# Expert layer: rows kept in token order, tiles gathered and scattered by row number on GpSimd

## What is computed

```python
# 1. banded attention, 8 heads of 64; keys: the first 8, and the last 96 up to the query
scores = q @ k.T / 8 - slope[h] * dist ;  a = softmax(scores where kept) ;  x = a @ v
# 2. one of 8 experts per token
logits = x @ w_gate ; gate = sigmoid(x @ w_local)
for s in tokens of a batch:
    e = argmax(logits[s]) if s == 0 or gate[s] < 0.5 else previous e
    out[s] = softmax(logits[s])[e] * (relu(x[s] @ w1[e]) @ w2[e])   # w1[e] 512x1024, w2[e] 1024x512
# 3. rotation and mixing
theta = x @ w_theta ; zr, zi = x * cos(theta), x * sin(theta)
u = x + w_tok_r @ zr + w_tok_i @ zi ;  result = u + relu(u @ w_ch)
```

## Time and profile before

| what | us |
|---|---|
| median of three executions | 620.63 |
| lowest and highest | 617.61 and 622.44 |
| the profiled execution | 617.87 |
| its span, first to last instruction | 616.2 |
| share of the span that TensorE is busy | 85% |
| mean granted TensorE clock | 0.934 of full speed |

### The profile page before, as it was taken

One profiled execution on the slowest core, in us unless ns is written; L12 is line 12 of the kernel. 1 busy time (PEld: TensorE's weight loads), 2 busy tenths in 40 slices (PEclk: granted clock), 3 DMA queues, 4 the chain that ended last, 5 costly groups with the idle time before them and its releaser, 6 DMA issues.

```text
span 616.2 us, 9126 instructions
## 1 busy us (share of the span) xinstructions
PE 522.7 (85%) x3252; PEld 430.0 (70%) x3253; DVE 282.8 (46%) x606; ACT 202.6 (33%) x420; POOL 116.4 (19%) x116
## 2 busy tenths in 40 slices
PE   0788888887502999999998999984799999999987
PEld 0566666664202999989997988973578887888866
DVE  5456565552332214141425144114789768655234
ACT  1466657651120113131334133113454423232011
POOL 4655555501043002020122020007100000000000
PEclk9998878898855999999999999996799999999999
DMA  5634434556023404572939564005200000000002
GB/s 196 219 127 137 132 131 133 173 248 277 1 106 132 170 34 182 227 286 106 374 104 398 247 238 171 34 26 152 61 0 2 1 1 1 17 18 18 35 34 87
DMA packets 22563, 77.61 MB, mean 126 GB/s; under 512 B 3456, under 2 KB 3712, under 8 KB 18432
## 3 DMA queue, kind: packets, MB, share of 16 engines
q0 software_dynamic: 8032, 46.67, 19.4%
q1 hardware_dynamic: 11904, 26.31, 12.8%
q10 hardware_dynamic: 2592, 4.20, 2.0%
HBM read 61.43 MB, written 15.73 MB: 125 GB/s over the span
## 4 chain that ended last, share of the span: by engine, by line
PE 59%; issue 17%; DVE 8%; DMA 6%; POOL 5%; ACT 3%; SPq 1%; DVEq 0%; POOLq 0%; ACTq 0%
PE ps L1154 33%; PE ps L1179 10%; POOL k_lo L452 4%; PE ps L998 3%; PE ps L1053 3%; PE ps L1037 3%; DMA q_raw<-in_q 3%; DMA w_sb<-in_w_experts 2%; PE ps L1115 2%; PE ps L1107 1%; POOL q_lo L447 1%; PE ps L1240 1%; PE ps L1018 1%; DVE w_lo L877 1%; PE ps L1165 1%
## 5 line engine op out<-in xcount | busy, mean ns | idle before, releaser
L1179 PEld LDWEIGHTS ps<-xT,w_sb 128*128 128x128 f32 x1024 | 118.0, 194 | 5.4 <-issue 3.0
L1179 PE MATMUL ps<-xT,w_sb 128*128 128x128 f32 x1024 | 118.5, 277 | 3.2 <-DMA w_sb<-in_w_experts 2.2
L868 DVE SCALAR_TENSOR_TENSOR hT_lo<-ps,hT_hi 128x512 fp32r<-128x512 f32 x32 | 21.8, 689 | 97.8 <-ACT hT_hi L576 97.6
L877 DVE TENSOR_TENSOR w_lo<-w_sb,w_hi 128x1024 fp32r<-128x1024 f32 x32 | 37.0, 1220 | 47.4 <-ACT w_hi L589 47.4
L1154 PE MATMUL ps<-w_hi,hT_hi 128*128 128x512 f32 x128 | 51.4, 401 | 2.2 <-DVE hT_lo L868 2.2
L525 ACT ACTIVATE prob<-raw,row_min 128x256 f32<-128x256 f32 (+1 forms) x96 | 46.0, 483 | 18.7 <-DVE row_min L736 18.6
L1154 PE MATMUL ps<-w_hi,hT_lo 128*128 128x512 f32 x128 | 50.0, 391 | 0.0
L1154 PE MATMUL ps<-w_lo,hT_hi 128*128 128x512 f32 x128 | 49.9, 390 | 0.0
L998 PE MATMUL ps<-k_hi,q_hi 64*128 64x256 f32 (+1 forms) x96 | 21.5, 441 | 31.5 <-POOL k_lo L452 30.1
L464 POOL DMA_DIRECT2D w_sb<-in_w_experts x32 | 17.3, 543 | 159.9 <-PE ps L1154 141.2
L576 ACT ACTIVATE hT_hi<-ps 128x512 fp32r<-128x512 f32 x32 | 19.0, 595 | 84.6 <-PE ps L1179 84.6
(11 more groups left out here) (184 smaller groups left out, 1009.0 us busy)
## 6 DMA issues: line engine op xcount, KB each, us to landing
w_sb<-in_w_experts POOLq DMA_DIRECT2D x32, 1024.0 KB, 9.1
v_sb<-in_vx SPq DMA_DIRECT2D x8, 640.0 KB, 5.1
slots<-zero SPq DMA_DIRECT2D x20, 256.0 KB, 5.2
xin<-slots SPq DMA_DIRECT2D x17, 256.0 KB, 2.6
slots<-yout ACTq DMA_DIRECT2D x16, 256.0 KB, 2.7
k_raw<-in_kx SPq DMA_DIRECT2D x8, 432.0 KB, 6.1
q_raw<-in_q SPq DMA_DIRECT2D x8, 384.0 KB, 6.5
out_x<-o_sb SPq DMA_DIRECT2D x12, 256.0 KB, 2.0
```

The source lines that it names most:

```text
L868: dve.scalar_tensor_tensor(hT_lo[:, part, :], ps[:, 1 + half, :].rearrange("p (c q) -> p c q", c=4), 0.0, hT_hi[:, part, :].bitcast(F32), ...
L877: dve.tensor_tensor(quarter(w_lo, par, q), quarter(w_sb, par, q), w2_hi_quarter(q).bitcast(F32), ALU.subtract).then_inc(s_w2_lo, 1)
L1179: last = pe.matmul(ps[:, 1 + half, f * P:(f + 1) * P], w_sb[:, par, c // 2, j:j + P], xT[:, c, :], start=(c == 0), stop=(c == DC - 1))
```

## The change

`slots` and its zero fill are gone. The tokens are stored in `x_rows` in token order, by two plain stores on SP as soon as attention is through. From the slots, VectorE and TensorE build the inverse map `token_at`: for each tile, one row number per partition (an out-of-range number where no token stands, which the DMA leaves out). GpSimd gathers each tile's rows from `x_rows` by these numbers, and scatters each result tile to `y_rows`. The loads of weights move from GpSimd's queue to SP's, ScalarE's store goes to GpSimd as a scatter, and the last gather becomes 12 plain loads on SP.

```diff
-                for t in (2 * h, 2 * h + 1):
-                    sp.dma_start(slots[t], zero[:]).then_inc(s_zero_out, 16)
...
+            sp.wait_ge(s_x_done, 1)
+            expert_weights(0, 0)
+            sp.wait_ge(s_x_done, PAIRS // GROUP)
+            for b in range(B):
+                sp.dma_start(x_rows.rearrange("(b i p) d -> b p i d", b=B, p=P)[b],
+                             x_tok[:, b * QT:(b + 1) * QT, :]).then_inc(s_x_out, 16)
+            expert_weights(1, 1)
...
+            with sp.Fori(0, E // 2 - 1) as pair:
+                for par in range(2):
+                    done = sp.value_load(first_tile[0:1, bass.ds(2 * pair + par + 1, 1)], min_val=1,
+                                         max_val=SLOT_TILES)
+                    sp.wait_ge(s_m_y, done + 1)
+                    expert_weights(2 * pair + par + 2, par)
...
-            with sp.Fori(0, total) as t:
-                sp.wait_ge(s_m_tx, t + 1)
-                sp.dma_start(xin[:], slots[bass.ds(t + 1, 1)].rearrange("o p d -> p (o d)")).then_inc(s_m_xin, 16)
+            sp.wait_ge(s_m_yout, 16 * total)
+            for n in range(NT):
+                sp.dma_start(x_tok[:, n, :], y_rows[n * P:(n + 1) * P, :]).then_inc(gathered[n], 16)
...
+            def rows_of(t):
+                pool.tensor_copy(rows_in[:], token_at[:, bass.ds(t + 1, 1)]).then_inc(s_row_in, 1)
+                pool.wait_ge(s_row_in, t + 1)
+                pool.sem_inc(s_row_seen, 1)
+                pool.indirect_dma_start(xin[:], None, x_rows, bass.IndirectOffsetOnAxis(ap=rows_in[:], axis=0),
+                                        bounds_check=last_row, oob_is_err=False).then_inc(s_m_xin, 16)
+
+            def store_rows(t):
+                pool.wait_ge(s_m_yev, t + 2)
+                pool.tensor_copy(rows_out[:], token_at[:, bass.ds(t + 1, 1)]).then_inc(s_row_out, 1)
+                pool.wait_ge(s_row_out, t + 1)
+                pool.sem_inc(s_row_seen, 1)
+                pool.indirect_dma_start(y_rows, bass.IndirectOffsetOnAxis(ap=rows_out[:], axis=0), yout[:], None,
+                                        bounds_check=last_row, oob_is_err=False).then_inc(s_m_yout, 16)
+
+            rows_of(0)
+            pool.wait_ge(s_m_tx, 1)
+            rows_of(1)
+            store_rows(0)
+            with pool.Fori(1, total) as t:
+                pool.wait_ge(s_m_tx, t + 1)
+                rows_of(t + 1)
+                pool.wait_ge(s_m_yout, 16 * t)
+                pool.sem_inc(s_y_free, 1)
+                store_rows(t)
...
                 act.wait_ge(s_m_y, t + 2)
-                act.wait_ge(s_m_yout, 16 * t + 16)
+                act.wait_ge(s_y_free, t + 1)
                 act.copy(yout[:], ps[:, 3, :]).then_inc(s_m_yev, 1)
-                act.wait_ge(s_m_yev, t + 2)
-                act.dma_start(slots[bass.ds(t, 1)].rearrange("o p d -> p (o d)"), yout[:]).then_inc(s_m_yout, 16)
...
-            dve.tensor_copy(slot[:], val).then_inc(s_slot_ready, 1)
+            then(dve.tensor_copy(slot[:], val))
+            dve.tensor_scalar(slot_part[:, 0, :], slot[:], 7, None, ALU.arith_shift_right).then_inc(s_slot_ready, 1)
+            then(dve.tensor_scalar(slot_part[:, 1, :], slot[:], P - 1, None, ALU.bitwise_and))
+            then(dve.tensor_copy(part_f[:], slot_part[:]))
...
+            dve.tensor_tensor(in_tile[:], con("tile").rearrange("p (n c) -> p n c", n=NT), along(part_f[:, 0, :], MAP),
+                              ALU.is_equal)
+            then(dve.tensor_tensor(at_place[:], over("place", P), along(part_f[:, 1, :], P), ALU.is_equal))
+            dve.tensor_tensor(of_tile[:], in_tile[:], along(con("token"), MAP), ALU.mult).then_inc(s_of_tile, 1)
...
+            dve.wait_ge(s_inverse, 1)
+            then(dve.tensor_scalar(found[:, 0, :], ps[:, 3, 0:MAP], 0.0, float(2 * TOKENS), ALU.is_equal, ALU.mult))
+            then(dve.scalar_tensor_tensor(found[:, 1, :], ps[:, 3, 0:MAP], 1.0, found[:, 0, :], ALU.subtract, ALU.add))
+            dve.tensor_copy(token_at[:, 1:], found[:, 1, :]).then_inc(s_map, 1)
...
+            for n in range(NT):
+                last = pe.matmul(ps[:, 3, 0:MAP], at_place[:, n, :], of_tile[:, n, :], start=(n == 0), stop=(n == NT - 1))
+            last.then_inc(s_inverse, 1)
```

More of the change, by code:

```diff
@@ L35 @@
 SLOT_TILES = (B * S - E) // P + E
+TOKENS = B * S
+MAP = SLOT_TILES + 1
 HALF = S // 2
@@ L56 @@
 _WIDTHS = [("rel", REL), ("key", S), ("ident", P), ("before", P), ("ones", P), ("first", NT), ("erev", NT * E), ("eone", NT * E), ("starts", E * NT),
-           ("carry", E * NT)]
+           ("carry", E * NT), ("place", P), ("token", NT), ("tile", NT * MAP)]
 COL, _at = {}, 0
@@ L82, in constants @@
     put("carry", np.tile(np.arange(NT) > 0, E)[None])
+    put("place", np.arange(P)[None])
+    put("token", p + np.arange(NT)[None] * P + 1)
+    put("tile", np.tile(np.arange(MAP), NT)[None])
     return t
@@ L128, in program @@
             consts, out):
-    slots = nc.dram_tensor("slots", [SLOT_TILES + 1, P, D], F32, kind="Internal").ap()
+    x_rows = nc.dram_tensor("x_rows", [TOKENS, D], F32, kind="Internal").ap()
+    y_rows = nc.dram_tensor("y_rows", [TOKENS, D], F32, kind="Internal").ap()
     with ExitStack() as ctx:
@@ L193, in program @@
         s_slot_ready = sem("slot_ready")
-        s_scattered = sem("scattered")
+        s_x_out = sem("x_out")
+        s_cleared = sem("cleared")
+        s_of_tile = sem("of_tile")
+        s_inverse = sem("inverse")
+        s_map = sem("map")
+        s_row_in = sem("row_in")
+        s_row_out = sem("row_out")
+        s_row_seen = sem("row_seen")
+        s_y_free = sem("y_free")
         s_m_xin = sem("m_xin")
@@ L253, in program @@
         half_pi = sb("half_pi", [P, 1])
-        slot = sb("slot", [P, NT], U32)
+        slot = sb("slot", [P, NT], I32)
+        token_at = sb("token_at", [P, 1 + MAP], U32)
+        rows_in = sb("rows_in", [P, 1], U32)
+        rows_out = sb("rows_out", [P, 1], U32)
         first_tile = sb("first_tile", [P, E + 1], I32)
@@ L299, in program @@
         small = sb("small", [P, 6, E])
+        slot_part = sb("slot_part", [P, 2, NT], I32)
+        part_f = sb("part_f", [P, 2, NT])
+        at_place = sb("at_place", [P, NT, P], F32R)
+        in_tile = sb("in_tile", [P, NT, MAP])
+        of_tile = sb("of_tile", [P, NT, MAP], F32R)
+        found = sb("found", [P, 2, MAP])
         end_routing = cursor[0]
@@ L411, in _ @@
                                  consts[:, key + WINDOW:key + S]).then_inc(s_rest_in, 16)
-                    sp.wait_ge(s_zeroed, 1)
-                for t in (2 * h, 2 * h + 1):
-                    sp.dma_start(slots[t], zero[:]).then_inc(s_zero_out, 16)
-            for t in range(2 * H, SLOT_TILES + 1):
-                sp.dma_start(slots[t], zero[:]).then_inc(s_zero_out, 16)
-            sp.wait_ge(s_slot_ready, 1)
-            total = sp.value_load(first_tile[0:1, E:E + 1], min_val=E, max_val=SLOT_TILES)
@@ L420, in _, with expert_weights @@
-            sp.wait_ge(s_scattered, 16 * NT)
-            sp.dma_start(xin[:], slots[0]).then_inc(s_m_xin, 16)
-            with sp.Fori(0, total) as t:
-                sp.wait_ge(s_m_tx, t + 1)
-                sp.dma_start(xin[:], slots[bass.ds(t + 1, 1)].rearrange("o p d -> p (o d)")).then_inc(s_m_xin, 16)
-            sp.wait_ge(s_m_yout, 16 * total + 16)
-            sp.sem_inc(s_y_stored, 1)
+            def expert_weights(e, par):
+                for piece in range(4):
+                    sp.dma_start(w_sb[:, par, piece, :], w_experts[bass.ds(4 * e + piece, 1)].rearrange(
+                        "o p c -> p (o c)")).then_inc(w_in[par], 16)
@@ new lines, in _ @@
+            sp.wait_ge(s_x_done, 1)
[5 more added lines that the diff above has]
+            expert_weights(1, 1)
+            sp.wait_ge(s_m_xin, 32)
+            sp.dma_start(wth[:], w_theta.rearrange("(c p) d -> p c d", p=P)).then_inc(s_wth_in, 16)
+            sp.dma_start(wch[:], w_ch.rearrange("(c p) d -> p c d", p=P)).then_inc(s_wch_in, 16)
@@ new lines, in _ @@
+            with sp.Fori(0, E // 2 - 1) as pair:
[4 more added lines that the diff above has]
+                    expert_weights(2 * pair + par + 2, par)
+                    for to, weights_t, loaded in ((wtr, w_tok_rT, s_wtr_in), (wti, w_tok_iT, s_wti_in)):
+                        sp.dma_start(to[:, bass.ds(2 * pair + par, 1), :], weights_t.rearrange(
+                            "(c p) t -> p c t", p=P)[:, bass.ds(2 * pair + par, 1), :]).then_inc(loaded, 16)
@@ L454, in _ @@
                 if h == 0:
-                    pool.memset(zero[:], 0.0).then_inc(s_zeroed, 1)
                     pool.wait_ge(s_mask, 2)
@@ L460, in _ @@
                     pool.tensor_scalar(levels[:, h + 1], levels[:, h], SLOPE_RATIO, None, ALU.mult).then_inc(s_level, 1)
[L462 to L469, removed]
@@ L470, in _ @@
-            pool.wait_ge(s_x_done, PAIRS // GROUP)
[L471 to L497, removed]
+            pool.wait_ge(s_x_done, PAIRS // GROUP)
```

(8 more changed lines are left out.)

12 lines of the change are left out of this document (6 added, 6 removed).

## The result

The changed kernel takes 659.3 us (median of 4, 656.8 to 660.2) against 619.5 before: ratio 1.063, 95% interval 1.058 to 1.069. I had said 639 and slower. The direction is right; the size, 39.8 us, is twice the 19.1 that the sum gave, and the time is inside the range of 610 to 664 only by its far end. The profiled execution took 659.25, with a span of 657.4, 41.2 more than before: 43.9 more in the expert loop, 3.7 more in what lies ahead of the slots, 1.1 more in the mixing layer, 7.3 less between the slots and the first transposes, 0.2 less after the loop.

What follows compares the result with a forecast made beforehand. TensorE was taken to bound the expert loop. Terms -7.9 ahead, -1.2 attention, -0.5 after and +28.7 in the loop gave +19.1 us, 639.7 from the median 620.63; forecast 639 us, range 610 to 664.

Steps and rivals of the forecast that it cites:

- the first rival: The gather lands before Y + 6.85 and TensorE never waits: 9.6 us gained outside the loop, about 4 inside; 607 us, chance 0.2.
- Ahead of the loop: From the slots to the first transposes: scatters and load go, map and gather come; minus 7.9 us (bounds 6 and 9).
- After the loop: Result scatters land about 1.2 us later, plain loads on SP pay that back; minus 0.5 us taken.
- The loop: Expert loop: gather issued too late, plus low clock, less two vanished waits for weights; plus 28.7 us.
- GpSimd's steps to the gather, no VectorE in the way: Expert loop, from the end of the `yout` copy: row-number copies, semaphores, scatter and DMA starts; gather issued at Y + 2.45.
- VectorE's two-input operations: Expert's first tile: row-number copy and gather each may wait for a w2 split operation; 1.3 us together (bounds 0 and 2.3).
- more, under the weights: Six first tiles: gather slowed by weights in flight, scaled from a plain load's 4.4 by packets; 2.4 us (bounds 1.3, 4.4).
- low clock, per tile: First tiles with weights: after a gap of 2.9 us TensorE runs at half clock for a while, costing 2.0 us.
- The 0.55 for the split of w2: Expert's first tile: the split of w2 holds its matmuls, so the gather's limit is about Y + 6.85, not Y + 6.3.
- Attention: Without the zero stores the second head's loads go out about 10 us sooner; small gain, minus 1.2 us.
- late, but short of a clock drop: Gather costs no more than a plain load, 1.9 us late in six tiles, no low clock; 620 us, chance 0.2.
- Late in every tile: Gather takes 4.6 us or the bounds check lengthens it, so ordinary tiles are about 1 us late too; 658 us, chance 0.15.

Runs made afterwards that it cites:

- weights held back: Changed kernel, but SP sends the next weights only when the gather needed in that tile has landed; 651.1 us, loop 249.4.
- the PSUM variant: Changed kernel, but VectorE's split of w2 takes one input from PSUM in place of SBUF (low part of w2 wrong); 649.0 us, loop 250.4.

## Why the prediction was right and wrong

**The bound, and the rank of the steps: right.** TensorE bounds the loop, the gather behind `store_rows` comes too late in six tiles, ordinary tiles are just in time (waits of 0.2 us in two of them), and the clock takes more on top. Putting the gather ahead takes all of it away. The loop is then 3.9 us shorter than before, which is the 4 that the first rival had put for a gather in time.

**Ahead of the loop: right.** 7.3 us against 7.9. The map took about what the steps say: the 12 matmuls 2.75 against 3.2, the gather 3.75 against 3.6.

**After the loop: right.** From the last `yout` copy to the first theta matmul it is 9.9 us against 10.1, so 0.2 gained and not 0.5.

**The loop: right in mechanism, wrong in size, +43.9 against +28.7.** The six tiles cost 41.5 us by the spacing of their `yout` copies: waits of 5.3 and low clock of 2.4 each, 46.2 together over a plain tile, less the 4.7 that the same tiles lost before. The terms, the first four for arrival of the gather after Y:

| term | said | measured | shown by |
|---|---|---|---|
| GpSimd's steps to the gather, no VectorE in the way | 2.45 | 3.2 | chain after; GpSimd idle 0.82 between each copy and its DMA |
| VectorE's two-input operations | 1.3 | 1.0 | gather start at Y + 4.2 against 3.2; the PSUM variant |
| gather alone | 3.6 | 3.4 | weights held back |
| more, under the weights | 2.4 | 4.2 (7.3 to 8.0 in all, mean 7.6) | six gathers of the changed kernel |
| arrival of the gather | 9.75 | 11.8 | sum of the four |
| low clock, per tile | 2.0 | 2.4 | spacing of the six copies less wait and plain tile |

The step that failed is the term "4.4 more, with 9 packets per DMA engine; a gather has 5, so 2.4 more". It measured 4.2, so the sum was short by 1.8 us in each of six tiles, and by some low clock behind it. The bounds that I gave for it did hold it, at the upper end, but the sum took the scaled value without a row that showed such scaling. The row of the plain load was also taken at another place: 7.0 us into the weights' load, where the gather is issued 4.5 in. How late in that load a gather is issued changes its time by about as much as the term was wrong (7.6 on average at 4.5 in, 5.6 to 6.2 us at 9.8 in). Between these two places a gather 7 us in would take about 6.7 us, an estimate, 3.3 more than alone against the plain load's 4.4. So fewer packets may have bought something after all; no run changes only them, and the weights leave from another queue than before. How much of the miss is the scaling and how much the place stays open.

The scatter in front isn't the main reason either: without one the gather took 8.4, of which 0.9 is VectorE's.

The second failed term is GpSimd's steps, 3.2 us where I had 2.45. I put 0.3 us ahead of an indirect DMA from DMAs that followed each other, and one that waits for a copy of its own row numbers has 0.8, twice in each chain. These two terms made the wait of TensorE 5.3 us on average (31.7 over six), where 9.75 against transposes at Y + 6.3 gave 3.45. The 0.55 for the split of w2 held: before, these tiles lost 0.6 us each to it, and now nothing. That the time is still inside the range is due to wide bounds, not to the sum.

**Attention: wrong sign, and its cause stays open.** I said -1.2 and the slots came 3.7 us later. The step itself held: the second head's first scores came 1.7 us sooner. What ran behind it was slower by more. Attention by stretch, before and then after:

```profile
30.00:140.00 110.00, 94.37 (x802) 67.23 (x801) 62.04 (x246) 66.12 (x214) 52.07 (x35) 0.88 0.45 152
```

```profile
30.00:140.00 110.00, 96.44 (x781) 68.86 (x777) 59.27 (x238) 65.41 (x213) 47.60 (x29) 0.80 0.31 113
```

PEclk was 0.80 and not 0.88, and VectorE got 238 operations done and not 246. But kernels with this very attention code gave slots at 172.2, 173.7, 174.0, 177.1, 178.7, 179.2, 180.6 and 184.4. The mean clock of the same stretch goes with it: 0.77 where the slots came at 184.4, 0.84 at 172.2, 0.85 at 174.0, 0.87 at 173.7. The gaps of 2 us at each head change are answered by a clock drop in some executions and not in others, and the stage moves by 12 us with it. Three of the eight were sooner than the 175.1 of the kernel before, at a mean clock no higher than its 0.88, so the forecast gain isn't refuted by the 3.7. With one profile of the kernel before, I can't say whether the change makes such drops likelier or the draw was a worse one. The same goes for the 1.1 us that the mixing layer took longer.

**The rivals.** "The gather is in time" and "late, but short of a clock drop" are out. "Late in every tile" named the right time, 658, for a wrong reason: ordinary tiles lost 1.6 us in all. In every tile behind the first, and in all runs that have both, an indirect DMA issued at the start of VectorE's split was held up (1.91 to 1.95 us and not 1.02 to 1.05), and the variant with one input in PSUM freed it. The Trainium skill, GPSIMD Engine Reference, Key points, says that GpSimd shares its SBUF interfaces with VectorE and contends with its instructions that have two SBUF inputs; the trace agrees. The gather took 3.4 us alone and 7.3 or more beside the weights in the changed kernel. The Trainium skill, DMA: Bandwidth & Descriptors, Anatomy of one DMA, gives a DMA from GpSimd about 2.0 us and its bytes over 436e3, 2.6 us for this one by that estimate; here the measurement decides.

## What to carry to other kernels

- When a transfer moves into another engine's program, ask which wait it now stands behind, and compare the moment at which it can be issued with the moment of its use. A transfer with 13 us of cover was put behind an eviction that left it 6; one line's place in the order was worth 48 us in the loop.
- Price a transfer that must land beside bulk loads by rows seen beside such loads, issued at the same place in them, and don't scale it down by its packets without a row that shows it. A gap that it makes on TensorE costs its length and then some of the work behind it at half clock.
- An engine's small steps between dependent instructions need their own row: here two of them, 0.8 us each, stood in every chain.

## What the hardware showed that I had not expected

- A gather of 256 KB takes 3.4 us from start to landing alone. Beside 4.75 MB of weights it takes 7.3 to 8.0 when issued 4.5 us after the first weight DMA and 5.6 to 6.2 when issued 9.8 us after it. A plain load of as many bytes takes 2.6 alone and 6.7 to 7.2 when issued 7.0 to 8.4 us after it.
- An indirect DMA on GpSimd takes 1.0 us. Under VectorE's split, operations of 1.2 us with two SBUF inputs, it took longer by about what was left of the operation then running: 0.9 us with 1.0 left (1.91 to 1.95 in all), 0.2 with 0.3 left (1.21). With one of the inputs in PSUM, 1.02.
- GpSimd is idle 0.8 us between the copy that makes row numbers and the indirect DMA that reads them, and 0.3 between indirect DMAs that don't depend on one.
- In the expert loop every gap of TensorE of 2.9 us and more was followed by a lower granted clock, in all these kernels. Of three gaps between 2.5 and 2.8 us one was (2.50, PEclk 0.69 behind it) and two were not (2.52 and 2.74, 1.00). The clock took 14.7 us of the changed kernel's 43.9.
